# Rebuilding the start of a fused attention and mixture-of-experts kernel, and feeding its rank products in fp32r

## The reference, cut to what matters

```python
for t in range(S):                                   # attention, S = 768
    cur = einsum('bhd,bhe->bhde', u[None] * kt, vt)
    y[:, :, t] = einsum('bhd,bhde->bhe', rt, state + cur)
    state = wt[:, :, :, None] * state + einsum('bhd,bhe->bhde', kt, vt)
...
xn = x / (norm(x) + 1e-06); en = expert_emb / (norm(expert_emb) + 1e-06)
logits = xn @ en.T / tau; expert_idx = argmax(logits, axis=1)      # first mixture
out[mask] = gate_w[mask, None] * (relu(x[mask] @ w1[e]) @ w2[e])
...
logits = x @ w_gate; e_idx = argmax(logits, axis=1)                # second mixture
out[mask] = gate_w[mask, None] * eom[mask, e, None] * ye
```

## Time and profile before

| | us |
|---|---|
| median of three runs | 836.56 |
| the three runs | 835.13, 837.51, 836.56 |
| profiled execution | 833.41 |
| its span in the trace | 831.7 |
| first scan of unit 0 (L719) starts | 23.08 |
| first product of the attention (L1069) starts | 27.70 |
| attention's last chunk routed (L821) | 198.49 |
| first mixture's loop on PE, from its first transposes | 211.54 to 536.7 |
| second mixture, from its first transposes | 544.09 to the end |

### The profile page before, as it was taken

The page is one execution under the profiler, slowest core; times in us unless marked ns, Lnnn a source line. Parts: engine busy times, 40 slices in busy tenths (PEclk is TensorE's granted clock), DMA queues, the critical chain, the costliest instruction groups (busy, mean ns, idle before and its releaser), DMA issues.

```text
span 831.7 us, 21488 instructions
## 1 busy us (share of the span) xinstructions
PE 740.6 (89%) x5583; PEld 653.1 (79%) x5584; DVE 504.0 (61%) x1357; ACT 390.4 (47%) x760; POOL 155.7 (19%) x197
## 2 busy tenths in 40 slices
PE   0689999982699999999999999569999999999994
PEld 0578777872588889898889888559999999999993
DVE  3989999986375574665575755535536263436621
ACT  1456676873254453544454544124525253425520
POOL 2344655554000000000000000100001100001100
PEclk9999999996799999999999999869999999999997
DMA  3366678744553342332343533125425151515110
GB/s 61 115 161 157 177 219 244 208 119 145 192 180 101 106 138 88 107 113 96 107 128 100 188 101 107 49 88 190 145 84 185 48 189 35 186 43 185 47 33 25
DMA packets 50269, 103.75 MB, mean 125 GB/s; under 512 B 7921, under 2 KB 29904, under 8 KB 50224
## 3 DMA queue, kind: packets, MB, share of 16 engines
q1 hardware_dynamic: 30080, 67.77, 26.0%
q10 hardware_dynamic: 15024, 21.17, 9.3%
q0 software_dynamic: 5120, 14.26, 4.8%
HBM read 85.73 MB, written 19.01 MB: 126 GB/s over the span
## 4 chain that ended last, share of the span: by engine, by line
PE 70%; DVE 10%; issue 7%; ACT 4%; ACTq 2%; DMA 2%; SPq 2%; POOL 1%; POOLq 0%; DVEq 0%
PE bank L1257 18%; PE bank L1283 17%; PE bank L1291 10%; PE bank L1262 9%; PE bank L1272 5%; PE bank L1246 2%; PE bank L1224 2%; DVE SF L728 2%; DVE Q L719 2%; ACT wall L532 2%; PE bank L1080 1%; PE bank L1143 1%; DVE Kb L733 1%; POOL rkp L378 1%; PE bank L1165 1%
## 5 line engine op out<-in xcount | busy, mean ns | idle before, releaser
L1257 PE MATMUL bank<-wall,xT_hi 128*128 (+1 forms) x660 | 180.6, 409 | 3.8 <-ACT xT_hi L621 3.8
L1283 PE MATMUL bank<-wall,hT_hi 128*128 x880 | 167.2, 341 | 0.7 <-ACT hT_hi L630 0.5
L1283 PEld LDWEIGHTS bank<-wall,hT_hi 128*128 128x128 f32 x880 | 154.5, 189 | 8.2 <-issue 5.8
L828 DVE TENSOR_TENSOR wall<-raw,wall 128x1024 f32 (+1 forms) x96 | 112.0, 1221 | 61.3 <-ACT wall L532 58.1
L1257 PEld LDWEIGHTS bank<-wall,xT_hi 128*128 128x128 f32 x660 | 120.2, 193 | 24.9 <-issue 3.5
L625 ACT ACTIVATE hs<-bank 128x512 f32<-128x512 f32 x110 | 65.0, 591 | 112.9 <-PE bank L1262 105.7
L532 ACT ACTIVATE wall<-raw 128x1024 f32 (+1 forms) x96 | 95.0, 1049 | 41.1 <-issue 41.1
L630 ACT ACTIVATE hT_hi<-bank 128x512 fp32r<-128x512 f32 x110 | 59.7, 595 | 77.9 <-PE bank L1272 77.9
L1262 PE MATMUL bank<-wall,xT_lo 128*128 (+1 forms) x330 | 95.6, 398 | 0.0
L1291 PE MATMUL bank<-wall,hT_lo 128*128 x440 | 91.1, 348 | 0.0
L447 POOL DMA_INDIRECT sorted<-yrow,slot x28 | 27.2, 972 | 308.3 <-DVE yrow L970 308.3
(11 more groups left out here) (192 smaller groups left out, 978.0 us busy)
## 6 DMA issues: line engine op xcount, KB each, us to landing
raw<-wall_in SPq DMA_DIRECT2D x96, 512.0 KB, 3.8
xin<-sorted ACTq DMA_DIRECT2D x59, 194.0 KB
rk<-rk_in SPq DMA_DIRECT2D x48, 192.0 KB
wb<-w_in SPq DMA_DIRECT2D x48, 96.0 KB
v_in<-v_src ACTq DMA_DIRECT2D x24, 192.0 KB
vT<-vT_in ACTq DMA_DIRECT2D x48, 96.0 KB
sorted<-padrow SPq DMA_DIRECT2D x16, 194.0 KB, 2.1
sorted<-yrow,slot POOLq DMA_INDIRECT x28, 2.6
```

The costliest lines, as they stand in the source:

```text
L828: v.tensor_tensor(w_lo[:, slot, cols], raw[:, q], w_hi[:, slot, cols].bitcast(F32), ALU.subtract).then_inc(w_split, 1)
L1257: pe.matmul(bank[n][:, :], xT_hi[:, k, :], w[:, bass.ds(slot, 1), cols].rearrange("p o n -> p (o n)"), start=(k == 0 and w is w_hi), stop= ...
L1283: pe.matmul(bank[2][:, 0:DM], hT_hi[:, j, :], w[:, bass.ds(slot, 1), W2 + j * DM:W2 + (j + 1) * DM].rearrange("p o n -> p (o n)"), start=( ...
```

## The change

Four things are changed.

1. DVE clears one buffer of `wb` and `rk` at a time and adds to `dve_const` after each. `vT`, `rtW1` and `emb` are cleared by POOL. SP loads the lower half of the partitions of units 0 and 1, ACT the upper half, each as soon as the buffer is clear.
2. The two loads of `u_in` stand between unit 0's and unit 1's on SP, with a semaphore `u_loaded` of their own; the other small loads come after unit 1's. DVE widens `u` after `pre(0)`. ACT takes the norms of the embeddings after unit 0's copies, and DVE makes the router's scale in unit 2's step. PE no longer waits for that scale at the start; the first reader of each value waits for it.
3. `before_r` and `ones_r` are fp32r copies of the matrices, and the one-hot choices and the running counts (`oh5`, `oha`) are written as fp32r, so the rank products of both routings are fp32r products. The offset of an expert's slots, before in one partition as `ecap`, is spread over the 128 partitions as `accbase`.
4. In `place1` the sum of the choices goes to an f32 tile `placed` first, and a copy takes it to the other half of `oh5`, after the slots are written.

```diff
-            sp.wait_ge(dve_const, 1)
-            load_unit(0, 0)
-            load_unit(0, 1)
+            def first_half(b):
+                sp.wait_ge(dve_const, b + 1)
+                sp.dma_start(wb[0:D, b, 0:SEG]..., w_in[0:1, b, 0]...).then_inc(rkw_in[b], 16)
+                sp.dma_start(rk[0:D, b]..., rk_in[0:1, b, 0]...).then_inc(rkw_in[b], 16)
+
+            first_half(0)
             for hf in range(2):
-                sp.dma_start(u_in[hf * HALF:hf * HALF + D, :], upair_in[hf]).then_inc(small_in, 16)
+                sp.dma_start(u_in[hf * HALF:hf * HALF + D, :], upair_in[hf]).then_inc(u_loaded, 16)
+            first_half(1)
+            sp.wait_ge(gp_const, 3)
+            for hf in range(2):
                 sp.dma_start(rtW1[hf * HALF:hf * HALF + D, :, 0:E], epair_in[hf]).then_inc(small_in, 16)
...
+            link(gp.memset(negone[:, :], -1.0))
+            gp.memset(negrange[:, :], -WRANGE * WRANGE).then_inc(gp_const, 1)
+            link(gp.memset(vT[:, :, :, :], 0.0))
+            link(gp.memset(rtW1[:, :, :], 0.0))
+            gp.memset(emb[:, :], 0.0).then_inc(gp_const, 1)
...
+            link(gp.tensor_copy(ones_r[:, :], ones[:, :]))
+            link(gp.tensor_copy(before_r[:, :], before[:, :]))
...
-            act.wait_ge(small_in, 160)
-            act.activation(embs[:, :], emb[:, :], ACT.Square, accum_out=en[:, 0:1]).then_inc(e_sq, 1)
-            act.wait_ge(e_sq, 1)
-            act.activation(en[:, 1:2], en[:, 0:1], ACT.Sqrt).then_inc(e_root, 1)
-            act.wait_ge(gp_const, 2)
+            def norms_of_experts():
+                act.wait_ge(small_in, 128)
+                ... (the same two activations)
+            def second_half(b):
+                act.wait_ge(dve_const, b + 1)
+                act.dma_start(wb[HALF:HALF + D, b, 0:SEG]..., w_in[0:1, b, 1]...).then_inc(rkw_in[b], 16)
+                act.dma_start(rk[HALF:HALF + D, b]..., rk_in[0:1, b, 1]...).then_inc(rkw_in[b], 16)
...
                 copy_a(u, b)
                 copy_kt(u, b)
-
-            act.wait_ge(dve_const, 1)
+                norms_of_experts()
+
+            second_half(0)
+            second_half(1)
+            act.wait_ge(gp_const, 3)
             load_v(0, 0)
             load_v(0, 1)
...
+            def clear(i):
+                link(v.memset(wb[:, i, :], 1.0))
+                link(v.memset(wb[:, i, 0:SEG].rearrange("p (a t) -> p a t", t=C1)[:, :, 0], 0.0))
+                v.memset(rk[:, i], 0.0).then_inc(dve_const, 1)
+                link(v.memset(wb[:, i, SEG:], 0.0))
...
                 if u == 0:
                     spread(0, 0, 0)
+                if u == 2:
+                    scale_of_experts()
...
-                v.reduce_sum(oh5[:, 1 - n % 2, 0], oh5[:, n % 2].rearrange("p b e -> p e b"), AXX)
+                v.reduce_sum(placed[:, :], oh5[:, n % 2].bitcast(F32).rearrange("p b e -> p e b"), AXX).then_inc(rt["base"], 1)
...
                 v.tensor_copy(slot4[:, q], at).then_inc(rt["slots"], 1)
+                v.wait_ge(rt["base"], n + 1)
+                v.tensor_copy(oh5[:, 1 - n % 2, 0], placed[:, :])
...
-            pe.wait_ge(e_ready, 1)
...
-                pe.matmul(RANKS, before[:, :], OH[:, E:], start=True, stop=False, skip_group_check=True)
+                pe.matmul(RANKS, before_r[:, :], OH[:, E:], start=True, stop=False, skip_group_check=True)
...
-                pe.matmul(bank[3][:, 32:32 + E], before[:, :], ohr, start=True, stop=False)
-                last = pe.matmul(bank[3][:, 32:32 + E], ones[:, :], acc, start=False, stop=True)
+                pe.matmul(bank[3][:, 32:32 + E], before_r[:, :], ohr, start=True, stop=False)
+                last = pe.matmul(bank[3][:, 32:32 + E], ones_r[:, :], acc, start=False, stop=True)
```

## The result

| | us |
|---|---|
| before, median on this chip | 835.85 |
| the changed kernel, median of four runs | 812.95 (811.39 to 813.74) |
| ratio, with its 95% interval | 0.9716 (0.9685 to 0.9746) |
| profiled execution of the changed kernel, and its span | 813.74, 812.0 |

The change takes 22.9 us off; 21.1 were forecast. On two more chips the same kernel took 816.4 (before: 835.25) and 815.63 (before: 835.13), 18.9 and 19.5 us less.

What follows compares the result with a forecast made beforehand. DVE bounds the attention, PE the first mixture's loop, after a single-file prologue. Terms -15.1 + 0.5 + 0.9 - 0.9 - 5.9 - 0.6 = -21.1 us take the median from 836.56 to 815.5; band 813.5 to 817.5, range 812.0 to 823.0.

Steps and rivals of the forecast that it cites:

- The start: Prologue: unit 0's scan starts at 8.0 (7.6 to 9.3) instead of 23.08, a gain of 15.1 us.
- The widening: DVE's stream between `pre(0)` and `pre(1)`: widening `u` adds 0.5 us, not hidden.
- The scale: Nine DVE steps, 1.6 us, ahead of unit 4's scan: cost 0 while the wait for unit 4's load stays.
- the norms: ACT's 2.1 us ahead of unit 1's `AT`: `AT` late by about 0.1, `KT` less, cost 0.
- 1.2 us of wait left ahead of unit 4: Attention: DVE still waits about 1.2 us before unit 4's scan, with the scale's nine steps ahead of it.
- The bound of +1.7 for long `vT` issues: ACT's early loads: two slow pairs make ACT 2.9 us late; bounds 0 and +1.7, 0 taken.
- rival (b): Start gives back some 3 us: unit 0 lands at 9.3, unit 2 late or scale shows; 818.5 us, chance 0.22.
- The halving: Rank products: fp32r needs one record instead of two, saving 0.22 us a tile, 5.9 us in the first mixture's loop.
- The attention's wait: Attention's end: with six records instead of twelve, DVE's 0.88 us wait for the totals goes, -0.9 us.
- The last four products: Last call of `before`: DVE's 1.19 us wait for its four products halves, -0.6 us.
- `place1`'s copy: Eight columns more copied for each chunk; five chunks in the DVE-bound part at 0.18 us, +0.9 us.
- rival (c): More than forecast: scan at 7.6 and shorter ranks help the attention by 2.8 us; 812.3 us, chance 0.11.

Runs made afterwards that it cites:

- scale_first: Changed kernel with the norms and the router's scale back ahead of unit 0's scan, loads in the new order: 825.98 us, ratio 0.987.
- small_first: Changed kernel with SP's eight small loads back ahead of its halves of units 0 and 1: 821.43 us, ratio 0.9809.
- rkp_after_widen: Changed kernel, but POOL's product rkp of unit 0 waits until the two copies that widen u have ended: 812.22 us, ratio 0.9704.
- no_scale: Changed kernel with seven of the nine steps of the router's scale left out ahead of unit 4: 805.55 us, ratio 0.9632.
- check_and_widen2: Changed kernel with POOL's rkp of unit 0 behind the widening copies and unit 2's range test ahead of ACT's loads, second run: 810.96 us, ratio 0.9691.

## Why the prediction was right, and where it was not

**The start.** 8.58 against 8.0, inside 7.6 to 9.3. The two terms were right in kind (DVE's clears and the landing), and the landing was the later by 1.1 to 1.4 us. The prediction had the clears end at 7.6; they ended at 7.2. What was not seen is how much of the gain hangs on the order of bytes rather than of instructions (scale_first, small_first). The smallest load's 1.9 us to its reader, from the earlier trace rows, held for DMA engines with little to do (busy 0.14 from 16 to 17 in the kernel before); behind some 1.9 MB of other loads it was 4.5.

**The widening.** Mis-sized: 0.5 forecast, 1.62 measured. The row of 0.54 us had been taken while POOL was idle; moved between `pre(0)` and `pre(1)`, the copy stands directly beside POOL's first product. rkp_after_widen shows it. What the forecast had just as little is that unit 1's products then ran clear of POOL and gave back 0.87 us, so unit 2's scan is 0.79 later behind unit 0's than before, not 1.66.

**The scale, the norms, ACT's loads.** The scale at nothing was right (no_scale), though it took 1.91 us and not 1.6. The prediction wanted 1.2 us of wait left ahead of unit 4; the profiles show none, 0.22 and 1.73. Unit 4's scan came at 33.19 (33.3 by the prediction's own sum, where it says 33.4), at 33.42 and at 35.24. The bound of +1.7 for long `vT` issues came true in part: unit 2's took 1.26, 1.57 and 2.95 us in three profiles of this kernel, and with the last, unit 4's scan stood 2.05 us later than in the first. So of rival (b) ACT's lateness came, at unit 4 and not at unit 2; unit 0's landing at 9.3 did not. The bound itself was added up wrongly: of 2.9 us with 1.2 + 0.3 absorbed, 1.4 are left, not 1.7. The norms ended at 20.83, 0.5 us after PE's product for unit 1's `AT`; behind it ACT waited 0.47 us for PE again, so they cost nothing that shows.

**The rank products.** The halving was right (one record of 0.11 us where there were two). The loop gained 8.2 us between the first tile and the last in the first profile, 5.9 forecast. 25 tiles at 0.25 are 6.2. The other 2.0 are in the last two tiles, 16.1 us together instead of 18.2, and 1.6 of them are the fall of the clock that this profile lacks in the last tile. That part is luck: nine of the twelve fp32r profiles have the fall. The attention's wait went as forecast, 0.88. The last four products gave 0.3 at `padi`, not 0.6. `place1`'s copy takes 0.16, as the row said, but each `place1` grew by 0.07 only, so the five cost some 0.4 us and not 0.9.

**What cancelled.** In the first profile the attention took 3.85 us more between the first scan and the last slots (+0.5 forecast). The widening is not the cause: from unit 0's scan to unit 4's the changed kernel is 0.22 us the shorter. Two late `rk` loads (1.77) and one fall of the clock (about 2.4) are. The loop and the last ranks took 2.0 less than forecast, 1.6 of it by the missing fall, and the start gave 0.6 less. 19.7 us of span came of it, against 21.1. So the terms for the start, the ranks and the scale were right in kind, while the nearness of this total owes something to falls of the clock that lie on both sides.

The medians, -22.9, -18.9 and -19.5 on three chips, lie on both sides of the forecast. On the first chip the median, 812.95, lies near rival (c)'s 812.3 and not in the forecast's band, but (c)'s mechanism did not come: the scan was at 8.58 and not 7.6, and no row shows the shorter ranks helping the attention before its end. Where the first chip's additional 3 us come from stays open; the kernel's own profiled execution, 813.74, was the slowest of its four runs.

## What to carry to other kernels

Load what the first instruction of the critical engine needs ahead of everything else, and count bytes in front of a load, not only issue slots: behind full DMA engines a small load reached its reader 4.5 us after its issue here, against 1.9. When a step is moved, look at what the other engines do at its new place, since its price was measured at the old one; and look at what it gets out of the way of there. Before a gain of a microsecond or two is put down to an edit, compare the granted clock of both profiles at that place: one fall in the last tile was worth 1.6 us here. After a gain at the start, follow the next load in the chain (here unit 4's) back to what its issuer waits for: a range test moved ahead of an issue brought unit 4's scan 1.6 us forward.

## What the runs showed of the hardware

- A DVE copy of 192 columns took 1.35 us beside a POOL product of two SBUF operands, about 0.27 without it. A DVE step of one column with two operands, L744, took 0.45, 0.62 and 0.45 us in the three profiles of the changed kernel and 0.21 us in check_and_widen2; POOL was at work on `AT` in each, so what sets it apart isn't settled.
- DVE's products `Rq` and `Kb` (128x512, two SBUF operands) took 1.12 and 1.11 us where they ran beside POOL's select on `AT` and 0.69 where they did not; POOL's two selects took 1.67 us beside the pair and 1.22 alone.
- The issue of two `vT` loads on ACT took between 0.92 and 2.95 us. The pair of 2.95 started with the DMA engines busy 0.92 in the microsecond before, but pairs of 0.92 us also stand beside busy engines (that at 9.39 in the changed kernel's start). What decides isn't settled.
- The granted clock fell to the 1.2 GHz level inside the attention in seven of fourteen profiles, of f32 and fp32r kernels alike, for 3.4 to 6.8 us. What a fall costs depends on the place: nothing between 147.7 and 154.5 in the changed kernel, 1 to 2 us behind unit 4's scan, about 2.4 us behind unit 23's, 1.6 us in the last tile of the first mixture's loop. In the second profile of the changed kernel the fall at 40.8 followed 3.45 us in which PE was idle; rkp_after_widen had 3.05 us of idle PE there and no fall (granted clock 1.00 from 40 to 60). What decides it stays open.
